# One-core linear attention, routed experts and a three-way maximum layer: the gate moved to the output's eviction, first row tiles transposed through two banks, filler matmuls at two boundaries, and the order of two products of the keys' norm

## The chip, the cores and the metric

The kernel runs on one core of one Trainium2 chip. The metric is the device time of one execution in microseconds (us); lower is better. The engines are TensorE (PE in the profile, with PEld for its weight loads), VectorE (DVE), ScalarE (ACT), GpSimd (POOL) and SyncE (SP, which here only starts DMAs).

## The reference

Three computations follow one another. All arithmetic is fp32.

```python
# attention: q, k, v are (4, 8, 768, 48), beta is (4, 8, 768)
k_n = k / (norm(k) + 1e-6)
for t in range(S):
    y[:, :, t] = einsum('bhd,bhde->bhe', q[:, :, t], state)
    v_old = einsum('bhde,bhd->bhe', state, k_n[:, :, t])
    state = state + beta_t * einsum('bhd,bhe->bhde', k_n[:, :, t], v_t - v_old)
x = y.transpose(0, 2, 1, 3).reshape(3072, 384)
# experts: one of 8 per row
e_idx = argmax(x @ w_gate); gate_w = softmax value of the chosen expert
out[row] = gate_w * sigmoid(x @ w_output_gate)[e_idx] * (relu(x @ w1[e]) @ w2[e])
# last layer
h = maximum(maximum(x @ w1, x @ w2), x @ w3);  out = h @ w_out
```

The combined factor of a row (the softmax value times the sigmoid) is positive. The last layer has no bias, so a positive factor on a row of its input can be applied to that row of its output.

## The kernel before, in words

There are three blocks of code. Each ends in a barrier of all engines, so no instruction of the next block runs before every engine has finished the one before.

**Attention and router.** The sequence is cut into chunks of 64 positions. Two streams (`st` 0 and 1) run half a step apart, and one step (12 in all) takes each of them through a pair of chunks. An order written out by hand sets what every engine issues: a step has 16 slots, and `walk` goes through the slots and calls `chain` (the work that carries the state from chunk to chunk, and the routing), `inv` (the inverse of a triangular matrix, per chunk) and `norm` (the key norms of the step that comes next). The tables `CHAIN`, `INV`, `PRE` and `NORM` give the slots. Engines are in order; semaphores tie them together.

The norm of the next step's keys is a row of short DVE operations, the parts 1 and 3 to 8 of `norm` (L586 to L607). Part 8 writes the inverse norm `nrm` (L607). Part 9 (L620) then makes `beta_k`, beta times the inverse norm, in four products of 64x8. POOL makes the normed keys `kn` (L664) from the raw keys and the same inverse norm, and waits for `inv_norm`, which part 8 raises. Behind part 9, DVE comes to `place` (L575), the routing product that reads what TensorE wrote to the stream's `chain` bank. TensorE's next `ks` product (L420) writes to that bank, so it waits for `place` (its semaphore is `routed`).

**Experts.** Rows stand sorted by expert in `x_sorted`. For each tile of 128 rows, `transpose_x` (L849) turns the loaded rows, ACT takes the high part and DVE the low part of the result (each operand is split in two fp32r parts, and a product takes three matmuls, helper `three`, L794), and the hidden and output products follow. Results go to `y_sorted`. The first tile needs its rows by DMA, the transposes, the high and the low part before the first product.

**Last layer.** There are 6 steps of 4 tiles (512 rows). POOL gathers rows from `y_sorted` in the original order (`gather`, L1114). DVE multiplies each gathered tile by its gate (`scale`, L1209) into one of two `scaled` buffers. TensorE transposes it into `o_bank[0]` (L1139), ACT takes the high part (L1176), DVE the low part (L1213). Three hidden products per 128 hidden columns (helper `three`, L1081) go to `h_bank`; ACT and DVE take their maximum (L1180, L1219, L1222) and split it (L1184, L1224). Then the output product fills `o_bank[t % 2]`, ACT copies it out (L1195) and SP stores it. For all steps but the first, the transposes stand between the hidden products of the step before. The first four tiles are transposed before the first step, one after the other, each waiting for the low part of the tile before (`x_lo`).

Of the kernel before, what the change touches and what calls it, by code (L numbers as in the profile page):

```python
# [16 lines left out]
P = 128  # L17
# [86 lines left out]
def attention_and_router(nc, ctx, sems, kt_in, kh, qh, vh, bh, cf_in, ch_in, wr_in, cf, ch, wr, routing, xs, ys, weights, w1, w2):  # L104
# [138 lines left out]
    NORM = {1: [0], 2: [1], 3: [2, 10], 5: [3], 6: [4], 7: [5], 8: [6, 13], 9: [7, 8, 9], 14: [11], 15: [12]}  # L243
# [80 lines left out]
    def _(pe):  # L324
# [146 lines left out]
        pe.matmul(bank[0][0][:, 0:E], ones16, counted[:], start=True, stop=True, skip_group_check=True).then_inc(totals_done, 1)  # L471

# [184 lines left out]
    def _(pool):  # L657
        def inv(k, par, st, what, lv):
            b = beta[:, 0, 2 * k + st, :]
            if what == "kn":  # L660
                pool.wait_ge(inv_norm, k + 1)
# [73 lines left out]
def experts(nc, ctx, sems, cf, routing, gate, slots, xs, ys, weights, w1, w2, w_in, w_out):  # L735
# [108 lines left out]
    def _(pe):  # L844
# [46 lines left out]

        transpose_x(0)
# [136 lines left out]
def last_layer(nc, ctx, sems, cf, gate, slots, ys, weights, out):  # L1029
# [14 lines left out]
    scaled = [sb(f"scaled{i}", [P, X]) for i in range(2)]  # L1044
# [16 lines left out]
    scaled_ready = sem("scaled_ready")  # L1061
# [16 lines left out]
    def three(pe, out, a, b, first, last):  # L1078
# [3 lines left out]
        return ins  # L1082

# [24 lines left out]
    def _(pool):  # L1108
        def gather(n, first):
            for t in range(NT):  # L1110
                if not first:
                    pool.wait_ge(scaled_ready, NT * n - NT + t + 1)
                    pool.sem_inc(passed_pool, 1)
# [16 lines left out]
    def _(pe):  # L1130
        def transpose_x(n, t, now=None):

            pe.wait_ge(scaled_ready, NT * n + t + 1)
            if t > 0:
                pe.wait_ge(x_lo, NT * n + t)
            elif now is not None:
                pe.wait_ge(o_out, NT * now + 1)
            for c in range(KX):
                ins = pe.transpose(o_bank[0][:, P * c:P * c + P], scaled[t % 2][:, P * c:P * c + P], ident)  # L1139
            ins.then_inc(x_done, 1)  # L1140
# [24 lines left out]

        for t in range(NT):
            transpose_x(0, t)
        for split in weights.last_lo:
            pe.wait_ge(split, 1)
# [3 lines left out]
    def _(act):  # L1173
        def x_part(n, t, par):
            act.wait_ge(x_done, NT * n + t + 1)
            act.copy(xt[par][0][:, :, P * t:P * t + P], o_bank[0][:, 0:X].rearrange("p (c t) -> p c t", c=KX)).then_inc(x_hi, 1)  # L1176
# [9 lines left out]
        def body(n, m, par, more):  # L1186
# [5 lines left out]
            for t in range(NT):  # L1192
                act.wait_ge(o_done, NT * n + t + 1)
                act.wait_ge(o_sent[t % 2], 8 * (NT * n + t - t % 2) + 1)
                act.copy(o_sb[t % 2][:], o_bank[t % 2][:, 0:X]).then_inc(o_out, 1)  # L1195
# [8 lines left out]
    def _(dve):  # L1204
        def scale(n, t):
            dve.wait_ge(rows_got[t], 16 * n + 16)
            if not (isinstance(n, int) and n == 0 and t < 2):
                dve.wait_ge(x_done, NT * n + t - 1)
            dve.tensor_scalar(scaled[t % 2][:], rows[t][:], gate[:, bass.ds(NT * n + t, 1)], None, ALU.mult).then_inc(scaled_ready, 1)  # L1209
# [121 lines left out]
```

## Time and profile before

| | us |
|---|---|
| median of 3 runs | 1111.56 |
| lowest and highest | 1108.06, 1112.52 |
| the profiled execution, its own time | 1108.98 |
| its span in the trace | 1107.3 |
| TensorE busy | 1026.3 |
| DVE, ACT, POOL busy | 509.7, 366.9, 335.4 |

The profiled execution is one more run. Its span counts from the first to the last recorded instruction; 1.7 us of its own time lie around it. The attention block runs to about 497 us of the span, the experts to about 777, the last layer to the end. The profile also gives the clock that TensorE was granted in a stretch, as a share of 2.4 GHz: 1.00 is 2.4 GHz and 0.50 is 1.2 GHz.

### The profile page before, as it was taken

What the parts mean: (1) busy time and instruction counts of PE and PEld (TensorE: products, weight loads), DVE (VectorE), ACT (ScalarE), POOL (GpSimd) and SP (SyncE); (2) the same over time, 40 slices, a digit from 0 to 9 for tenths busy, and PEclk for the clock granted to TensorE, in tenths of its full rate; (3) what the DMA queues carried; (4) which work ended last, traced back from release to release, by engine and by line L of the source; (5) the groups of instructions that cost most, each with busy time, mean ns of one, the idle gap of its engine ahead of it and who ended that gap; (6) DMA issues with size and microseconds to landing.
All of it is one profiled execution on the core that took longest, in us unless ns stands there. A gap on an engine that the chain in (4) does not pass through costs nothing. (4 is left out here: it accounts for less than half of the span.)

```text
span 1107.3 us, 30948 instructions
## 1 busy us (share of the span) xinstructions
PE 1026.3 (93%) x13260; PEld 895.4 (81%) x13260; DVE 509.7 (46%) x1085; ACT 366.9 (33%) x731; POOL 335.4 (30%) x251
## 2 busy tenths in 40 slices
PE   4898999999999999849999999999599999999998
PEld 3787888887888778737999999998488888888888
DVE  5575665666666655435444444433332323233221
ACT  1455544554555455412222222221121222122111
POOL 3444253435233422115352555525310001000000
PEclk9999998999999999958999999999699999999999
DMA  9212112121212111044344444223201010100000
GB/s 313 110 34 65 55 53 60 55 72 41 72 58 70 41 44 34 9 151 162 102 155 165 171 165 171 86 86 114 71 22 39 19 44 14 48 16 22 15 15 29
DMA packets 58056, 84.90 MB, mean 77 GB/s; under 512 B 28880, under 2 KB 52816, under 8 KB 55376
## 3 DMA queue, kind: packets, MB, share of 16 engines
q1 hardware_dynamic: 52272, 46.94, 13.5%
q0 software_dynamic: 5664, 36.18, 9.6%
q8 instruction: 98, 1.61, 0.6%
q14 instruction: 22, 0.18, 0.1%
HBM read 61.67 MB, written 21.43 MB: 75 GB/s over the span
## 5 line engine op out<-in xcount | busy, mean ns | idle before, releaser
L1081 PE MATMUL hb<-early,last_h 128*128 128x512 f32 x648 | 208.0, 402 | 1.2 <-DVE early L1213 1.2
L1081 PEld LDWEIGHTS hb<-early,last_h 128*128 128x128 f32 x648 | 121.7, 191 | 29.4 <-DVE early L1213 1.6
L1081 PE MATMUL hb<-early,last_l 128*128 128x512 f32 x324 | 129.3, 399 | 0.0
L1219 DVE TENSOR_TENSOR m<-hb,m 128x512 f32<-128x512 f32 x36 | 24.9, 692 | 132.3 <-PE hb L1081 132.3
L329 PEld LDWEIGHTS bank<-t,n_hi 64*64 64x64 f16 x2688 | 65.7, 111 | 23.6 <-issue 7.9
L540 DVE TENSOR_TENSOR p<-bank,cf 128x512 f16<-128x512 f32 x96 | 66.1, 689 | 32.2 <-PE bank L329 31.8
L329 PE MATMUL bank<-t,n_hi 64*64 64x64 f16 x2688 | 72.7, 195 | 4.9 <-issue 4.2
L1081 PE MATMUL ob<-wo_h,early 128*128 128x384 f32 x288 | 75.1, 339 | 0.0
L1081 PEld LDWEIGHTS hb<-early,last_l 128*128 128x128 f32 x324 | 61.6, 190 | 15.0
L1003 POOL TENSOR_TENSOR late<-w_raw,late 128x3072 fp32r<-128x3072 f32 x8 | 54.5, 6812 | 57.6 <-DVE late L943 57.3
L1114 POOL DMA_INDIRECT rows<-y_sorted,idx x24 | 23.0, 959 | 159.1 <-DVE scaled L1209 155.8
L537 DVE TENSOR_TENSOR t<-bank,cf 128x512 f16<-128x512 f32 x72 | 49.8, 692 | 45.7 <-PE bank L329 44.9
L912 ACT CAST ht_h<-ht_bank 128x512 fp32r<-128x512 f32 x56 | 32.9, 587 | 109.3 <-PE ht_bank L866 55.4
L489 ACT CAST t<-bank 128x512 f16<-128x512 f32 x96 | 56.3, 587 | 27.2 <-PE bank L329 25.0
L930 DVE TENSOR_TENSOR ht_l<-ht_bank,ht_h 128x512 fp32r<-128x512 f32 x56 | 38.7, 692 | 56.7 <-ACT ht_h L912 56.2
L794 PE MATMUL y_acc<-early,ht_h 128*128 128x384 f32 x240 | 63.8, 347 | 0.0
L794 PE MATMUL h_bank<-early,xt_h 128*128 128x512 f32 x180 | 58.5, 407 | 1.4 <-DVE xt_l L925 1.3
L420 PE MATMUL chain<-state,kq_t 128*128 128x96 f32 x384 | 54.8, 286 | 5.2 <-issue 5.0
L664 POOL TENSOR_TENSOR kn<-k_raw,nrm 128x384 f32<-128x384 f32 x24 | 20.1, 836 | 125.5 <-DVE nrm L607 125.2
L491 ACT CAST tt<-bank 128x512 f16<-128x512 f32 x96 | 57.0, 593 | 1.4 <-PE bank L329 1.3
L1003 POOL TENSOR_TENSOR early<-w_raw,early 128x3072 fp32r<-128x3072 f32 x6 | 40.9, 6810 | 52.7 <-DVE early L943 52.5
L794 PE MATMUL y_acc<-late,ht_h 128*128 128x384 f32 x208 | 55.2, 346 | 1.5 <-DVE ht_l L930 1.5
(163 smaller groups left out, 2194.7 us busy)
## 6 DMA issues: line engine op xcount, KB each, us to landing
w_raw<-w POOLq DMA_DIRECT2D x14, 1536.0 KB, 7.6
kq_t<-qh SPq DMA_DIRECT2D x24, 256.0 KB, 3.3
y_sorted<-y_sb SPq DMA_DIRECT2D x31, 192.0 KB, 1.9
x_in<-x_sorted SPq DMA_DIRECT2D x29, 192.0 KB, 2.8
k_raw<-kt_in SPq DMA_DIRECT2D x24, 192.0 KB, 3.2
v_in<-vh SPq DMA_DIRECT2D x24, 192.0 KB, 3.6
k_own<-kh SPq DMA_DIRECT2D x24, 192.0 KB, 3.4
out<-o_sb SPq DMA_DIRECT2D x24, 192.0 KB, 1.8
```

Of the source, the lines that this page charges most:

```text
L329: ins = pe.matmul(out[s, C * u:C * u + C], lhs(s, u), rhs(s, u), start=first and u == 0, stop=True, skip_group_check=True)
L420: ins = pe.matmul(out[:, W * p:W * p + W], kq_t[par][st][:, NP * e + p, :, :].rearrange("q a t -> q (a t)"), state[st][:, p].rearrange("q ...
L489: act.copy(t16[st][:], tb).then_inc(t_out[st], 1)
L491: act.copy(tt16[st][:], ttb).then_inc(tt_out[st], 1)
L537: dve.tensor_tensor(t16[st][:], pb, mask_of(None), ALU.mult).then_inc(jacobi_out[st], 1)
L540: dve.tensor_tensor(p16[st][:], pb, mask_of(lv), ALU.mult).then_inc(prod_out[st], 1)
L794: ins = pe.matmul(out, a[x], b[y], start=first and i == 0, stop=last and i == 2)
L912: act.copy(ht[0][:, 4 * n:4 * n + 4].rearrange("p c t -> p (c t)"), ht_bank[n][:, :]).then_inc(ht_hi[n], 1)
L930: dve.tensor_tensor(ht[1][:, 4 * n:4 * n + 4].rearrange("p c t -> p (c t)"), ht_bank[n][:, :], ht[0][:, 4 * n:4 * n + 4].rearrange("p c t ...
L1003: pool.tensor_tensor(splits[par][i][1], weights.flat_raw(i), splits[par][i][0], ALU.subtract).then_inc(weights.lo_ready[i], 1)
L1081: ins = pe.matmul(out, a[x], b[y], start=first and i == 0, stop=last and i == 2, skip_group_check=True)
L1219: dve.tensor_tensor(m1[f % 2][:], h_bank[f % 2][1][:, :], m0[f % 2][:], ALU.max).then_inc(m1_out, 1)
```

## The change

Four things change.

1. In the last layer, the gathered rows are transposed as they are. The gate is applied by DVE when it takes the output product out of its bank (`output`), in place of ACT's copy; `scale`, the `scaled` buffers and their semaphore are gone. POOL's next gather into a row buffer waits for the transposes of that buffer.
2. The first four tiles of the last layer are transposed through `o_bank[0]` and `o_bank[1]` in turn, so a tile waits for the low part of the tile two before it. The later tiles still use `o_bank[0]` alone.
3. TensorE gets matmuls whose results nobody reads: 12 of fp16 at the end of the attention block, 12 at the start of the experts, 12 at the start of the last layer and 3 after each of its first four transposed tiles. All have 512 columns.
4. In the attention, POOL's `kn` of every step but the first waits for `beta_k_ready` (raised by part 9) in place of `inv_norm`. The norm parts 3 to 9 stand one slot earlier in `NORM`.

```diff
-    NORM = {1: [0], 2: [1], 3: [2, 10], 5: [3], 6: [4], 7: [5], 8: [6, 13], 9: [7, 8, 9], 14: [11], 15: [12]}
+    NORM = {1: [0], 2: [1], 3: [2, 10], 4: [3], 5: [4], 6: [5], 7: [6], 8: [7, 8, 9, 13], 14: [11], 15: [12]}
...
         pe.matmul(bank[0][0][:, 0:E], ones16, counted[:], start=True, stop=True, skip_group_check=True).then_inc(totals_done, 1)
+        for _ in range(12):
+            pe.matmul(bank[1][2][:, :], tri16, flat(n_hi[1]), start=True, stop=True, skip_group_check=True)
...
             if what == "kn":
-                pool.wait_ge(inv_norm, k + 1)
+                if k >= 1:
+                    pool.wait_ge(beta_k_ready, k + 1)
+                else:
+                    pool.wait_ge(inv_norm, 1)
...
+        pe.wait_ge(weights.hi_ready[0], 1)
+        for _ in range(12):
+            pe.matmul(h_bank[1][:, :], w1s[0][0][:, 0, 0:P], w1s[0][0][:, 0, 0:512], start=True, stop=True, skip_group_check=True)
         transpose_x(0)
...
+    def x_bank(n, t):
+
+        return o_bank[t % 2 if isinstance(n, int) and n == 0 else 0]
...
-                    pool.wait_ge(scaled_ready, NT * n - NT + t + 1)
+                    pool.wait_ge(x_done, NT * n - NT + t + 1)
...
-            pe.wait_ge(scaled_ready, NT * n + t + 1)
-            if t > 0:
-                pe.wait_ge(x_lo, NT * n + t)
-            elif now is not None:
-                pe.wait_ge(o_out, NT * now + 1)
+            pe.wait_ge(rows_got[t], 16 * n + 16)
+            if now is None:
+                to = o_bank[t % 2]
+                if t >= 2:
+                    pe.wait_ge(x_lo, t - 1)
+            else:
+                to = o_bank[0]
+                if t > 0:
+                    pe.wait_ge(x_lo, NT * n + t)
+                else:
+                    pe.wait_ge(o_out, NT * now + 1)
             for c in range(KX):
-                ins = pe.transpose(o_bank[0][:, P * c:P * c + P], scaled[t % 2][:, P * c:P * c + P], ident)
+                ins = pe.transpose(to[:, P * c:P * c + P], rows[t][:, P * c:P * c + P], ident)
...
+        for split in weights.last_lo:
+            pe.wait_ge(split, 1)
+
+        def keep_warm(count):
+            for _ in range(count):
+                pe.matmul(h_bank[1][2][:, :], ws[0][0][:, 0, 0:P], ws[0][0][:, 0, 0:512], start=True, stop=True, skip_group_check=True)
+
+        keep_warm(12)
         for t in range(NT):
             transpose_x(0, t)
-        for split in weights.last_lo:
-            pe.wait_ge(split, 1)
+            keep_warm(3)
...
-            for t in range(NT):
-                act.wait_ge(o_done, NT * n + t + 1)
-                act.wait_ge(o_sent[t % 2], 8 * (NT * n + t - t % 2) + 1)
-                act.copy(o_sb[t % 2][:], o_bank[t % 2][:, 0:X]).then_inc(o_out, 1)
...
-        def scale(n, t):
-            dve.wait_ge(rows_got[t], 16 * n + 16)
-            if not (isinstance(n, int) and n == 0 and t < 2):
-                dve.wait_ge(x_done, NT * n + t - 1)
-            dve.tensor_scalar(scaled[t % 2][:], rows[t][:], gate[:, bass.ds(NT * n + t, 1)], None, ALU.mult).then_inc(scaled_ready, 1)
+        def output(n, t):
+            dve.wait_ge(o_done, NT * n + t + 1)
+            dve.wait_ge(o_sent[t % 2], 8 * (NT * n + t - t % 2) + 1)
+            dve.tensor_scalar(o_sb[t % 2][:], o_bank[t % 2][:, 0:X], gate[:, bass.ds(NT * n + t, 1)], None, ALU.mult).then_inc(o_out, 1)
...
             for f in range(KF):
-                if more and f < NT:
-                    scale(n + 1, f)
                 hidden(n, f)
                 if more and f < NT:
                     x_part(n + 1, f, 1 - par)
+            for t in range(NT):
+                output(n, t)
...
         for t in range(NT):
-            scale(0, t)
             x_part(0, t, 0)
```

## Rows read from the trace of the kernel before

**Rows 1.** The page: busy time of each engine; the last chain by line.
```profile
PE 1026.3 (93%) x13260; PEld 895.4 (81%) x13260; DVE 509.7 (46%) x1085; ACT 366.9 (33%) x731; POOL 335.4 (30%) x251
...
PE hb L1081 21%; PE ob L1081 7%; PE ob L1139 1%; DMA rows<-y_sorted,idx 0%; ACT early L1176 0%; DVE scaled L1209 0%; DVE early L1213 0%; ACT o_sb L1195 0%; POOL idx L1118 0%; POOLq L1302 0%
```

**Rows 2.** Windows: length, busy us (instructions) by engine, granted clock, DMA share, GB/s.
```profile
134.80:138.00 3.20, 3.20 (x47) 2.89 (x46) 2.86 (x12) 2.14 (x5) 0.84 (x2) 0.50 0.02 5
172.80:179.00 6.20, 6.20 (x102) 5.79 (x101) 3.75 (x16) 2.87 (x6) 2.33 (x4) 0.50 0.01 3
...
501.70:506.60 4.90, 4.90 (x12) 3.84 (x13) 3.15 (x10) 0.60 (x1) 0.78 (x1) 0.50 0.28 84
776.70:791.20 14.50, 3.60 (x12) 2.01 (x12) 3.94 (x12) 2.52 (x5) 7.99 (x10) 0.50 0.32 88
791.20:796.90 5.70, 5.66 (x13) 4.45 (x14) 2.89 (x2) 1.99 (x2) 2.17 (x3) 0.50 0.17 54
797.00:1104.50 307.50, 307.49 (x1452) 262.34 (x1450) 90.40 (x147) 62.27 (x114) 15.17 (x19) 1.00 0.08 25
```

**Rows 3.** Timeline of PE, attention: start, length, instruction, idle before and its releaser.
```profile
215.29 1.10 PE L420 MATMUL chain<-state,kq_t 128*128 128x96 f32 x8 [0.73 <-issue]
...
289.20 1.10 PE L420 MATMUL chain<-state,kq_t 128*128 128x96 f32 x8 [0.54 <-issue]
...
399.27 0.99 PE L420 MATMUL chain<-state,kq_t 128*128 128x96 f32 x7 [0.73 <-issue]
```

**Rows 4.** Timeline of DVE, the end of one step's norm.
```profile
249.37 0.17 DVE L598 TENSOR_TENSOR nrm<-nrm 128x16 f32<-128x16 f32 x1
...
249.78 0.25 DVE L607 RECIPROCAL nrm<-nrm 128x16 f32<-128x16 f32 x1
250.07 1.25 DVE L620 TENSOR_TENSOR beta_k<-nrm,beta 64x8 f32<-64x8 f32 x4
251.35 0.17 DVE L575 TENSOR_TENSOR place<-chain,chosen 128x8 f32<-128x8 f32 x1
```

**Rows 5.** Timeline, one step earlier, a narrow window: the second factor product, POOL's keys.
```profile
213.92 0.72 DVE L620 TENSOR_TENSOR beta_k<-nrm,beta 64x8 f32<-64x8 f32 x1
...
213.79 0.83 POOL L664 TENSOR_TENSOR kn<-k_raw,nrm 128x384 f32<-128x384 f32 x1 [11.46 <-DVE nrm L607]
```

**Rows 6.** Timelines of PE, DVE and SP at the first boundary.
```profile
490.71 0.17 PE L471 MATMUL bank<-counted,ch 128*128 128x8 f16 x1 [1.02 <-POOL counted L690]
499.54 0.90 PE L849 MATMUL xt_bank<-cf,x_in 128*128 128x128 f32 x3 [8.66 <-DMA x_in<-x_sorted]
...
497.26 0.38 DVE L989 MEMSET y_sb<- 128x384 f32 x1 [4.13 <-PEq L1297]
...
494.21 0.42 SPq L319 DMA_DIRECT2D x_sorted<-zeros  x1
```

**Rows 7.** The chain that ended last: two first groups of hidden products of the last layer.
```profile
791.24 9.12 PE hb L1081 x27
...
800.69 6.33 PE hb L1081 x27
```

**Rows 8.** Timelines of PE, DVE and POOL at the second boundary.
```profile
782.00 0.90 PE L1139 MATMUL ob<-cf,scaled 128*128 128x128 f32 x3 [7.92 <-DVE scaled L1209]
...
781.36 0.58 DVE L1209 TENSOR_SCALAR scaled<-rows,gate 128x384 f32<-128x384 f32 x1 [4.02 <-DMA rows<-y_sorted,idx]
...
782.07 0.95 POOL L1114 DMA_INDIRECT rows<-y_sorted,idx  x1 [0.30 <-issue]
785.48 0.19 POOL L1118 COPY idx<-slots 128x4 uint32 x1 [2.46 <-DMA rows<-y_sorted,idx]
```

**Rows 9.** Timelines: the last eviction, the nearest DVE eviction, DVE's idle in an output product.
```profile
1104.52 0.48 ACT L1195 COPY o_sb<-ob 128x384 f32<-128x384 f32 x1 [2.69 <-PE ob L1081]
...
774.21 0.56 DVE L936 COPY y_sb<-y_acc 128x384 f32<-128x384 f32 x1 [4.62 <-PE y_acc L794]
...
1058.15 0.69 DVE L1219 TENSOR_TENSOR m<-hb,m 128x512 f32<-128x512 f32 x1 [14.87 <-PE hb L1081]
```

More of the change, by code:

```diff
@@ L1043, in last_layer @@
     rows = [sb(f"rows{t}", [P, X]) for t in range(NT)]
-    scaled = [sb(f"scaled{i}", [P, X]) for i in range(2)]
     w1_early, w2_early = weights.split_early()
@@ L1060, in last_layer @@
     rows_got = [sem(f"rows_got{t}") for t in range(NT)]
-    scaled_ready = sem("scaled_ready")
     x_done = sem("x_done")
@@ L1175, in x_part @@
             act.wait_ge(x_done, NT * n + t + 1)
-            act.copy(xt[par][0][:, :, P * t:P * t + P], o_bank[0][:, 0:X].rearrange("p (c t) -> p c t", c=KX)).then_inc(x_hi, 1)
+            act.copy(xt[par][0][:, :, P * t:P * t + P], x_bank(n, t)[:, 0:X].rearrange("p (c t) -> p c t", c=KX)).then_inc(x_hi, 1)
         def hidden(n, f):
@@ L1204, in _ @@
     def _(dve):
-        def scale(n, t):
-            dve.wait_ge(rows_got[t], 16 * n + 16)
-            if not (isinstance(n, int) and n == 0 and t < 2):
-                dve.wait_ge(x_done, NT * n + t - 1)
-            dve.tensor_scalar(scaled[t % 2][:], rows[t][:], gate[:, bass.ds(NT * n + t, 1)], None, ALU.mult).then_inc(scaled_ready, 1)
+        def output(n, t):
+            dve.wait_ge(o_done, NT * n + t + 1)
+            dve.wait_ge(o_sent[t % 2], 8 * (NT * n + t - t % 2) + 1)
+            dve.tensor_scalar(o_sb[t % 2][:], o_bank[t % 2][:, 0:X], gate[:, bass.ds(NT * n + t, 1)], None, ALU.mult).then_inc(o_out, 1)
         def x_part(n, t, par):
             dve.wait_ge(x_hi, NT * n + t + 1)
-            dve.tensor_tensor(xt[par][1][:, :, P * t:P * t + P], o_bank[0][:, 0:X].rearrange("p (c t) -> p c t", c=KX),
+            dve.tensor_tensor(xt[par][1][:, :, P * t:P * t + P], x_bank(n, t)[:, 0:X].rearrange("p (c t) -> p c t", c=KX),
                               xt[par][0][:, :, P * t:P * t + P], ALU.subtract).then_inc(x_lo, 1)
```

## The prediction

> **What bounds the kernel now.** I read the page first. TensorE is busy 93% of the span and no other engine half of it, and the last chain is TensorE alone with small pieces of the last layer's start around it [rows 1]. So time can only come from TensorE's own idle stretches and from stretches in which it ran slowly. The windows show both. From 797.0 to 1104.5 TensorE has no gap and its clock is 1.00, so nothing in the body of the last layer can be gained by relieving another engine there; it can only be lost. At either boundary the clock is at 0.50 (1.2 GHz) and TensorE mostly waits; it comes back to 1.00 only after 4.9 us of unbroken products at the first boundary and 5.7 us at the second [rows 2]. Then I read TensorE's timeline in the attention for its idle times. One is regular: 0.73 us ahead of the `ks` product of stream 1, in six steps from 215.3 to 399.3 (five of 0.73, one of 0.54) [rows 3]. The DVE rows just ahead tell why: the tail of the norm, then the four `beta_k` products, then `place`, and `ks` starts about 0.1 us after `place` ends [rows 4]. The narrow window shows that the second `beta_k` product took 0.72 us and ended with POOL's `kn`, which had begun 0.13 us before it; the last three took 1.1 us together, so the two others 0.18 each [rows 4, 5].
>
> **The attention.** If `kn` starts only behind `beta_k`, the four products take 4 x 0.18 = 0.7 us and not 1.25, which brings `place` 0.55 us forward. Norm part 6 (0.17 us, 0.2 with its gap) leaves the stretch ahead of `place` for slot 7, where DVE has idle time: another 0.2. Parts 7 to 9 move over a slot in which DVE has nothing else, so their order on DVE is unchanged; parts 3 to 5 move into idle stretches between short PSUM reads. Together 0.75 us, against a wait of 0.73: the wait goes in all six steps, 5 x 0.73 + 0.54 = 4.2 us [rows 3, 4]. What is late next: the gram product waits for ACT's `kq_t`, which ends about when the shifted gram could start, and everything behind it follows TensorE. The added wait on POOL holds back `kn` by 0.7 us, and behind it the counting, the scatter of rows and the mask; `kn` is read only in the next slot 0, and POOL had been idle 11.5 us before it [rows 5], so this costs nothing. In the steps before 215 the wait is hidden under pauses of TensorE or under the slow clock. Bounds: 0, if another wait takes its place, to 5.7 us, if two earlier steps gain 0.73 as well. I take 4.2.
>
> Two stretches of the attention ran at 0.50 without being idle, 3.2 and 6.2 us long [rows 2]. At full clock they would have taken half, so they cost 1.6 + 3.1 = 4.7 us. Nothing in the change touches these places, and I cannot tell from one trace whether they come in every execution; they go into the range.
>
> **The first boundary.** The 12 fillers at the end of the attention start behind the 0.17 us product at 490.71. There is no row of a 128x512 fp16 matmul; the nearest are fp32r ones of this size, 12 in 4.9 us at the slow clock [rows 2] and 27 in 6.33 us, 0.234 each, at the full one [rows 7]. So the fillers run 490.9 to about 496.0 at the slow clock. SP issues the last DMA of the block at 494.21 and the experts start at 497.1 to 497.3 [rows 6], so that DMA's landing hides them, with about 1 us to spare. If they ran over, each would cost 0.41 us.
>
> The second 12 start at about 497.3. Before, TensorE's first transposes stood at 499.54, when the rows had come [rows 6], and the first product at 501.7. At the full clock the fillers take 2.8 us and end at 500.1; transposes of 0.5 (half of the 0.90 at the slow clock) and the high and low parts (1.1 with their gaps) bring the first product to 501.7, where it was, now at the full clock: a gain of half of 4.9, 2.4 us [rows 2]. At the slow clock they take 4.9 to 5.1, end at 502.4 and put the first product at 504.5, a loss of 2.8 us; with the clock back by then, 2.8 - 2.4 = 0.4 us of loss. Which one depends on when the clock rises. After 4.9 to 5.7 us of work, as in the two rows, it would rise at 495.8 to 496.6, right about when the first fillers end. I take the case that a third of the second batch is still slow (4 x 0.2 us late): -2.4 + 0.8 = -1.6 us, with bounds of -2.4 and +2.8.
>
> A rule of the Trainium skill bears on this. "TensorE: Matmul & The Clock Gate", section "HAM oscillation — how this bites in real kernels", says that bursts of matmuls with waits between them can meet the slow clock each time anew; the same page's Part 1 has the point of the rise vary from run to run. By it, two batches with 1.3 us between them need not hold the clock, and this boundary would be the loss of rival 2. The rows here have no two bursts of this length with such a gap, so they neither agree nor disagree.
>
> **The second boundary.** Before, the rows of the first tile came at 781.34, DVE scaled them, and then four tiles went one after the other through one bank; the first product stood at 791.24 [rows 7, 8]. From 782.00 that is 9.2 us. In the new order 12 fillers start at about 777.3, just when the clock has fallen, and end at about 782.3 (12 x 0.42); the clock has risen by then or shortly after (777.3 + 4.9 to 5.7). The rows are there, no scaling stands between, so the first transposes start at 782.3, not 782.0: 0.3 us later. Each tile then takes 0.5 for its transposes and 0.7 for three fillers: tile 1 at 783.5, tile 2 at 784.7 (its bank is free: the low part of tile 0 ends at 783.9), tile 3 at 785.9. The fourth gather is issued at 782.07 and POOL sees all four landed at 785.48 [rows 8], so tile 3 could not start before 785.4 anyhow. Its transposes, high and low part end at 787.5: the first product comes 3.7 us earlier. The last three fillers end at 787.1 and are hidden. The first 27 products took 9.12 us against 6.33 at the full clock [rows 7], another 2.8. Sum: -6.5 us. Bounds: -7.0 (tile 3 the moment it lands, at 785.4) and -3.0 (clock back only at 785: all four tiles slow, about 2 us later, and part of the 2.8 lost). I take -6.3. With the first product at 787.5, ACT's and DVE's split of `w_out` ends in time for the first maxima, as it stands behind the same parts as before.
>
> **The evictions.** The 24 `scale` products (0.41 to 0.58 us each) leave DVE and 24 evictions come in. The nearest row is DVE's copy of a 128x384 bank, 0.56 us against ACT's 0.48 [rows 9]. DVE idles 14.9 us between its last work of a step and the next [rows 9], and an output tile takes 12.7 / 4 = 3.2 us of TensorE with two banks in turn, so 0.56 us is hidden there and costs nothing; without that cover it would be 24 x 0.56 = 13.4 us. Only the last stands in the open: +0.1 us. POOL's gathers now wait for the transposes instead of the scaling, one product group later, with more than 20 us until the rows are used: nothing.
>
> **Sum.** -4.2 - 1.6 - 6.3 + 0.1 = -12.0 us. The profiled execution took 1108.98 in its own time (its span 1107.3 and 1.7 around it): 1097.0. It was 2.6 us faster than the median of the runs, 1111.56, so the same change from the median would be 1099.6. I take about the middle, 1098.
>
> **The rivals.**
> 1. In the attention another wait takes the place of the one removed, or `beta_k` is held by something else: 0 instead of -4.2. For it: a hand-made order with little slack, and ACT's `kq_t` right behind. Against it: the wait after `place` is 0.1 us, so it alone released `ks`. About 1102.
> 2. The first boundary turns to a loss, the second batch slow throughout: +1.5 instead of -1.6. About 1101.
> 3. At the second boundary the clock comes late: -3.0 instead of -6.3. About 1101.5.
> 4. Slower: DVE's eviction is exposed. DVE is in order, so if `output` holds up the maxima of the next step, or a bank comes free too late, TensorE waits each time. At 0.56 us for all 24 that is +13.4: 1.4 us over before, about 1112. It decides from 0.5 us exposed per eviction on. Against it stands the idle time of 14.9 us.
>
> **How the numbers follow.** The forecast as summed has a chance of 0.60, with a range of its own of 1094 to 1101 (the two slow stretches of the attention gone or doubled make most of it). Rival 1 has 0.13, rival 2 0.12, rival 3 0.11, rival 4 0.04. The range of 1091 to 1105 runs from the forecast without the slow stretches (1097.0 - 4.7 = 1092.3, less the 1 us of the bounds) to two rivals at once. A measurement of this kernel can tell about 0.5%, 5.6 us, from no change: that is 1106. Rivals 1 to 3 alone all stay below it. Two of them together with an unlucky execution, and most of rival 4, fall within it: 0.05. Slower, the rest of rival 4 (evictions longer than 0.56): 0.015. Faster: 0.935.
>
> **What would show it.** The attention: the four `beta_k` products at 0.7 us, `kn` starting behind them, and no idle time before L420 in the regular steps. The first boundary: the attention's last DMA, not TensorE, still ahead of the barrier; the clock at 1.00 when the first product starts, at 501.7 or a little later counted from the same barrier. The second: the transposes 1.2 us apart, the first product about 10.3 us after the barrier and not 14.1, 27 products in 6.33 us. The last layer: from the first product on as long as before, no gap on TensorE. A prediction too low would show TensorE waiting for `o_out` or `m2_out`, or fillers at 0.43 us right up to the first transposes of the experts.

## The result, and the profile after

The changed kernel takes 1096.72 us (median of 4 runs, 1095.28 to 1098.27). The kernel before, run in turn with it, takes 1109.81 us. The ratio is 0.989, with a 95% interval of 0.9856 to 0.9924: the kernel is 1.1% faster. The forecast was 1098.0, within 1091 to 1105.

The profiled execution of the changed kernel has a span of 1094.7 us, against 1107.3: 12.6 us less. Laid side by side, from mark to mark, the two profiled executions differ like this. A mark is the start of a row in a timeline of TensorE, or the end of a product; the start of a block is where DVE's first instruction behind the barrier stands.

| stretch | before, us | after, us | difference | predicted |
|---|---|---|---|---|
| start to the attention's last counting product (L471) | 490.71 | 486.93 | -3.78 | -4.2 |
| L471 to the end of the first expert tile's hidden products | 17.56 | 15.36 | -2.20 | -1.6 |
| from there to the experts' last product | 265.81 | 265.87 | +0.06 | 0 |
| to the start of the last layer's block | 3.12 | 3.12 | 0 | 0 |
| block start to the end of the first 27 hidden products | 23.16 | 16.28 | -6.88 | -6.3 |
| the rest of the last layer | 306.94 | 307.14 | +0.20 | +0.1 |

The page of the changed kernel, busy time and last chain, to lay beside [rows 1]:

```profile
PE 1034.8 (95%) x13308; PEld 899.7 (82%) x13308; DVE 507.0 (46%) x1085; ACT 355.3 (32%) x707; POOL 335.3 (31%) x251
...
PE hb L1087 21%; PE ob L1087 7%; PE ob L1155 1%; PE hb L1187 1%; DVE o_sb L1227 0%; DVE early L1231 0%; ACT early L1199 0%
```

ACT has lost 24 instructions and 11.6 us of work, TensorE has gained 48 matmuls and 8.5 us. Neither figure says where the time went; that is seen at the places themselves. First DVE's timeline at the end of a norm, and its last eviction. This answers to [rows 4, 9]:

```profile
322.55 0.25 DVE L609 RECIPROCAL nrm<-nrm 128x16 f32<-128x16 f32 x1
322.84 0.69 DVE L622 TENSOR_TENSOR beta_k<-nrm,beta 64x8 f32<-64x8 f32 x4
323.56 0.17 DVE L577 TENSOR_TENSOR place<-chain,chosen 128x8 f32<-128x8 f32 x1
...
357.96 0.25 DVE L609 RECIPROCAL nrm<-nrm 128x16 f32<-128x16 f32 x1
...
1091.72 0.62 DVE L1227 TENSOR_SCALAR o_sb<-ob,gate 128x384 f32<-128x384 f32 x1 [2.55 <-PE ob L1087]
```

The four `beta_k` products take 0.69 us where they took 1.25. The two reciprocals are one step apart: 35.41 us, where the same pair stood 36.17 apart. POOL's timeline, with `kn` behind `beta_k` (which, of that step, began at 215.38), the first of the four gathers, and the copy that waits for all four:

```profile
216.14 0.83 POOL L669 TENSOR_TENSOR kn<-k_raw,nrm 128x384 f32<-128x384 f32 x1 [11.41 <-DVE beta_k L622]
...
772.31 1.02 POOL L1124 DMA_INDIRECT rows<-y_sorted,idx  x1 [0.59 <-POOL idx L1128]
...
779.58 0.18 POOL L1128 COPY idx<-slots 128x4 uint32 x1 [2.48 <-DMA rows<-y_sorted,idx]
```

TensorE's timeline at the two boundaries, beside [rows 6, 8]:

```profile
486.93 0.17 PE L471 MATMUL bank<-counted,ch 128*128 128x8 f16 x1 [1.01 <-POOL counted L695]
486.96 4.85 PE L473 MATMUL bank<-n_hi,ch 128*128 128x512 f16 x12
493.38 2.98 PE L899 MATMUL h_bank<-early 128*128 128x512 f32 x12 [1.57 <-PEq L1314]
...
498.00 0.70 PE L799 MATMUL h_bank<-early,xt_h 128*128 128x512 f32 x2 [1.25 <-DVE xt_l L933]
...
771.40 4.46 PE L1187 MATMUL hb<-last_h 128*128 128x512 f32 x12 [3.24 <-PEq L1319]
775.70 0.49 PE L1155 MATMUL ob<-cf,rows 128*128 128x128 f32 x3
...
779.25 0.55 PE L1155 MATMUL ob<-cf,rows 128*128 128x128 f32 x3
```

The chain that ended last, with the first two groups of hidden products, beside [rows 7]:

```profile
780.96 6.60 PE hb L1087 x27
787.88 6.32 PE hb L1087 x27
```

And the windows, columns as in [rows 2]: the first expert tile, the start of the last layer in two parts, its body, and a stretch of the attention.

```profile
493.00:503.00 10.00, 8.37 (x40) 6.62 (x40) 5.75 (x17) 3.03 (x6) 0.87 (x1) 1.00 0.37 120
771.40:776.00 4.60, 4.60 (x16) 3.65 (x16) 0.03 (x2) 0.00 (x0) 3.12 (x4) 0.66 0.27 78
776.00:781.00 5.00, 4.53 (x24) 2.76 (x22) 2.23 (x4) 2.61 (x5) 1.48 (x3) 1.00 0.29 87
788.00:1092.00 304.00, 303.68 (x1434) 259.26 (x1432) 97.50 (x151) 51.13 (x91) 16.01 (x20) 1.00 0.08 26
139.50:150.00 10.50, 10.23 (x126) 9.00 (x127) 3.76 (x8) 2.69 (x6) 5.64 (x5) 0.51 0.18 51
```

The reader sees full clock throughout the first expert tile, the clock risen before the gathered rows are turned, and a last layer still without gaps. The last row is the one thing that has not changed: 10.5 us of the attention still run at half clock while TensorE is busy for 10.23 of them.

One caution goes ahead of all experiments. Eleven variants were run, and the changed kernel once more; each profile is one execution, and executions of one kernel lie far apart (the kernel before: 1101.6 to 1116.5 us over all its runs; the variants: 3 to 15 us from end to end). One execution of `b2_second_batch_only` (4951 us) and one of `d4_changed_again` (2467 us) took several times as long, for no reason on record; the ratios leave them out, and without the latter the median of `d4_changed_again` is 1097.83 us and not 1099.34. A part worth 2 us can't be told from the medians of whole runs. The ratios are given, but the verdicts are read from stretches between marks, which repeat far better: from the transposes that follow the first 27 hidden products (0.16 us ahead of their modelled end) to the end of the span, the last layer takes 307.2 to 307.3 us in every profile of the changed kernel's kind that keeps the evictions as they are.

### The profile page after: what moved, and what is told of

The parts are those of the page before. It is cut to its first block and busy times, and to the rows that moved or that the text cites. A ratio compares the mean times of both kernels' runs of the same rounds, so it can differ in the third digit from the quotient of the medians.

```text
span 1094.7 us, 30983 instructions
## 1 busy us (share of the span) xinstructions
PE 1034.8 (95%) x13308; PEld 899.7 (82%) x13308; DVE 507.0 (46%) x1085; ACT 355.3 (32%) x707; POOL 335.3 (31%) x251
## 3 DMA queue, kind: packets, MB, share of 16 engines
q0 software_dynamic: 5664, 36.18, 9.6%
## 5 line engine op out<-in xcount | busy, mean ns | idle before, releaser
L439 PE MATMUL chain<-z,n_kb_a 128*128 128x96 f32 x384 | 56.2, 291 | 1.1 <-issue 1.1
```

Source lines behind the costliest of these rows:

```text
L439: ins = pe.matmul(out[:, W * p:W * p + W], n_kb_a[par][st][:, NP * e + p, 1:3, :].rearrange("q a t -> q (a t)"), z[st][:, p].rearrange("q ...
```

## The experiments

Every variant below is an edit of the changed kernel.

### The attention: undone, and its two halves

`a1_attention_undone` puts the old table and the old wait back. `b1_slots_only` keeps the new table and puts back the wait alone.

```diff
-    NORM = {1: [0], 2: [1], 3: [2, 10], 4: [3], 5: [4], 6: [5], 7: [6], 8: [7, 8, 9, 13], 14: [11], 15: [12]}
+    NORM = {1: [0], 2: [1], 3: [2, 10], 5: [3], 6: [4], 7: [5], 8: [6, 13], 9: [7, 8, 9], 14: [11], 15: [12]}   # a1 only
...
             if what == "kn":
-                if k >= 1:
-                    pool.wait_ge(beta_k_ready, k + 1)
-                else:
-                    pool.wait_ge(inv_norm, 1)
+                pool.wait_ge(inv_norm, k + 1)                                                                  # a1 and b1
```

> The changed kernel with the attention edits alone taken back (the old slots of the norm, and the keys' product waiting for the inverse norm again). My theory (the factor products were held by POOL's key product, and the place product behind them released the next ks product): the four beta_k products take 1.25 us again, the idle time of 0.73 us ahead of the ks product is back in six steps, and the run is 3.8 to 4.2 us longer than the changed kernel, all of it before the product of the totals. Rival (the attention got shorter because fewer or shorter slow-clock stretches fell in it, not by the wait): the attention is as long as in the changed kernel once the time at the 0.50 clock is taken out, so 0 to 1 us.

> The changed kernel with the keys' product waiting for the inverse norm again, as before, and the new slots of the norm kept. The clean steps of the attention were 36.17 us long before and 35.41 with the change. My theory (0.55 us from the order against POOL, 0.2 from norm part 6 leaving the stretch): the beta_k products take 1.25 us, the clean steps 35.9 to 36.0 us, about 3 us more than the changed kernel over the steps in which it counts. Rival (the slots do it all, the products' length is hidden): 35.4 us per clean step, 0 us.

Measured: a1 takes 1099.4 us (4 runs), a ratio to the kernel before of 0.9897 (0.9851 to 0.9943); b1 1098.79 (10 runs), 0.9915 (0.9881 to 0.9948). DVE's timeline of a1:

```profile
325.26 0.25 DVE L609 RECIPROCAL nrm<-nrm 128x16 f32<-128x16 f32 x1
325.55 1.25 DVE L622 TENSOR_TENSOR beta_k<-nrm,beta 64x8 f32<-64x8 f32 x4
...
361.44 0.25 DVE L609 RECIPROCAL nrm<-nrm 128x16 f32<-128x16 f32 x1
```

DVE's and TensorE's timelines of b1:

```profile
322.98 0.25 DVE L609 RECIPROCAL nrm<-nrm 128x16 f32<-128x16 f32 x1
323.26 1.25 DVE L622 TENSOR_TENSOR beta_k<-nrm,beta 64x8 f32<-64x8 f32 x4
...
358.94 0.25 DVE L609 RECIPROCAL nrm<-nrm 128x16 f32<-128x16 f32 x1
...
360.78 0.99 PE L420 MATMUL chain<-state,kq_t 128*128 128x96 f32 x7 [0.50 <-issue]
```

The same kind of step takes 36.18 us in a1 (361.44 - 325.26), 35.96 in b1 and 35.41 in the changed kernel, which all three have in steps without a pause of TensorE. So the new slots bring 0.21 of the 0.76 and the order against POOL the other 0.55, the sizes the prediction gave them (0.2 and 0.55). `beta_k` goes back to 1.25 us whenever `kn` may start beside it. TensorE's wait ahead of L420 is 0.73, 0.50 and none. Summed over the attention, the idle time ahead of L420 was 5.0 us in the kernel before (9 times), 4.7 in a1 (8), 1.6 in the changed kernel (twice, 1.25 of it in one pause at 139.77) and 5.6 in b1 (11). So the wait in b1 is shorter but comes more often, and this sum doesn't rank the two halves; the length of a step does.

The whole stretch to L471 doesn't show this well. It was 486.93 us in the changed kernel's first profile, and with the same attention 481.00 to 494.14 in the profiles of other variants. The medians of a1 and of the changed kernel differ by 2.7 us in the right direction, inside their scatter, and not by the 3.8 to 4.2 that were expected. The rival's own measure doesn't decide either. With half of the time at the 0.50 clock taken out, the stretch to L471 is 475.6 us in a1 and 475.4 in the changed kernel, which is where the rival put it; but the same figure lies between 470.4 and 479.5 in the other profiles with the changed attention.

A shorter stretch tells more. The five steps between the reciprocals at 213.46 and 397.44 us of the kernel before take 183.98 us. They take 183.03 in a1, 181.16 in b1, 179.53 in the changed kernel, and 177.84 to 183.15 in the ten other profiles with its attention; the median of these eleven is 179.53. The forecast for them was 3.5 us less (five of the six waits, 4 x 0.73 + 0.54). The median is 3.5 below a1 and 4.5 below the kernel before, which is about that, and ten of the eleven lie below a1 and the kernel before. With one profile each of a1, b1 and the kernel before, it is not measured to a microsecond.

### The first boundary: no fillers, half of them, more of them

`a2_no_fillers_first` takes away both batches, `b2_second_batch_only` the first one; `d2_first_16` makes the first one 16; `d4_changed_again` is the changed kernel once more.

```diff
         pe.matmul(bank[0][0][:, 0:E], ones16, counted[:], start=True, stop=True, skip_group_check=True).then_inc(totals_done, 1)
-        for _ in range(12):                        # a2, b2: both lines gone; d2: range(16)
-            pe.matmul(bank[1][2][:, :], tri16, flat(n_hi[1]), start=True, stop=True, skip_group_check=True)
...
-        for _ in range(12):                        # a2: both lines gone
-            pe.matmul(h_bank[1][:, :], w1s[0][0][:, 0, 0:P], w1s[0][0][:, 0, 0:512], start=True, stop=True, skip_group_check=True)
         transpose_x(0)
```

> The changed kernel without both filler batches at the first boundary. My theory (the clock alone): from the totals product to the last hidden product of the first expert tile it takes 17.5 us as before the change, not 15.4; the clock comes back about 5 us after the first hidden product; +2.2 us in all. Rival (the gain at this boundary came from something else that moved earlier): 15.4 to 16 us without fillers too.

> The changed kernel without the first batch of 12 fillers, the second kept. My theory (a batch that starts at the 0.50 clock holds up the transposes by more than it gives back): the 12 fillers take 4.5 to 5 us, the first hidden product stands 13.0 to 13.6 us behind the totals product (11.1 in the changed kernel, 11.0 before), and the first expert tile's hidden products end after 17.3 to 17.9 us, as before the change: no gain at this boundary. Rival (the second batch alone carries the gain): 15.4 to 16.9 us.

> The changed kernel with 16 and not 12 fillers in the first batch. Theory (the clock rises under the first batch and falls again while TensorE waits for the barrier, if that wait is over about 2 us; four more fillers shorten it by 0.9 us): the second batch runs at the full clock, and the first tile's hidden products end 15.3 to 15.6 us behind the totals product, not 16.8 as in four of the six executions profiled so far. Rival (the fall does not hang on the length of the gap): 16.7 to 16.9 again.

> The changed kernel once more, for the scatter between executions beside the other three and a second profile. Expected: 1094 to 1100 us in the median; clean attention steps of 35.4 us; the first boundary 15.4 or 16.8 us; the second 9.6 to 9.7 us to the first product.

Measured: a2 1100.02 us (9 runs), ratio 0.9911 (0.9885 to 0.9938); b2 1101.39 (9 runs), 0.9937 (0.9907 to 0.9968); d2 1097.97 (6 runs), 0.9907 (0.987 to 0.9944); d4 1099.34 (6 runs), 0.9901 (0.9874 to 0.9928).

In a2 TensorE idles 9.17 us up to the transposes. TensorE's timeline of b2 and of d2, their batches:

```profile
499.00 4.74 PE L897 MATMUL h_bank<-early 128*128 128x512 f32 x12 [6.27 <-PEq L1312]
```

```profile
487.76 5.55 PE L473 MATMUL bank<-n_hi,ch 128*128 128x512 f16 x16
494.17 3.01 PE L899 MATMUL h_bank<-early 128*128 128x512 f32 x12 [0.86 <-PEq L1314]
```

TensorE's timeline of d4, which is the changed kernel unchanged:

```profile
494.14 0.17 PE L471 MATMUL bank<-counted,ch 128*128 128x8 f16 x1 [1.01 <-POOL counted L695]
494.17 4.44 PE L473 MATMUL bank<-n_hi,ch 128*128 128x512 f16 x12
500.58 4.58 PE L899 MATMUL h_bank<-early 128*128 128x512 f32 x12 [1.97 <-PEq L1314]
504.99 0.49 PE L854 MATMUL xt_bank<-cf,x_in 128*128 128x128 f32 x3
506.73 0.70 PE L799 MATMUL h_bank<-early,xt_h 128*128 128x512 f32 x2 [1.25 <-DVE xt_l L933]
```

Its windows over the second batch and behind it:

```profile
500.58:505.00 4.42, 4.42 (x13) 3.44 (x14) 1.38 (x5) 1.73 (x3) 0.00 (x0) 0.61 0.54 180
...
500.58:501.00 0.42, 0.42 (x2) 0.38 (x3) 0.32 (x2) 0.42 (x1) 0.00 (x0) 1.00 0.00 0
501.10:504.40 3.30, 3.30 (x9) 2.55 (x8) 0.96 (x4) 1.21 (x3) 0.00 (x0) 0.50 0.71 237
...
505.00:509.00 4.00, 2.75 (x14) 2.12 (x13) 2.19 (x11) 0.48 (x1) 0.00 (x0) 1.00 0.32 102
```

Here the second batch takes 4.58 us in place of 2.98. The granted clock was still 1.00 through the 1.97 us between the batches and for the first 0.4 us of the second one; then it was 0.50, and it was 1.00 again before the transposes. Eight profiles have the two batches of 12 (the variants that edit other places have them too). They fall in two groups, and the other counts stand beside them. The first three columns are lengths in us; the last is counted from L471.

| executions | first batch takes | idle before the second | second batch takes | end of the first tile's hidden products |
|---|---|---|---|---|
| 12 and 12: after, b1, d3 | 4.85 to 5.28 | 1.14 to 1.57 | 2.98 to 3.01 | 15.32 to 15.39 |
| 12 and 12: a1, a3, a4, c1, d4 | 4.04 to 4.47 | 1.94 to 2.38 | 4.4 to 4.6 | 16.73 to 16.90 |
| 16 and 12: d2 | 5.55 | 0.86 | 3.01 | 15.54 |
| 0 and 12: b2 | | 6.27 | 4.74 | 17.05 |
| none: before, a2 | | | | 17.56, 18.35 |

The second batch starts 6.43 to 6.44 us behind L471 in all eight. So a first batch that meets an early rise of the clock is over sooner, the idle time behind it is longer, and the second batch is slow: the clock fell 0.2 to 0.4 us before it began in a1 and a3, and 0.3 to 0.5 us after in a4, c1 and d4. Even then the stretch is 0.7 to 0.8 us shorter than it was in the kernel before (and about 1.5 shorter than in a2), because the clock is back for the first real products. Both batches at their best bring 2.2.

Two of these expectations were not met, and a third proves little. a2 was to take 17.5 us and took 18.35; its transposes wait 0.5 us longer for their rows than in the kernel before, and the rest is a later rise of the clock. So two single profiles without fillers lie 0.8 us apart, and every gain against either has that uncertainty. b2, at 17.05, lies between its two theories (17.3 to 17.9, and 15.4 to 16.9): the second batch alone is worth 0.5 us against the kernel before and 1.3 against a2, which is not settled. d2 came out as its theory said (15.54), but three of the eight profiles with 12 fillers did as well, so one profile does not show that 16 are better.

### The second boundary: no fillers, one bank

```diff
-        keep_warm(12)                              # a3
         for t in range(NT):
             transpose_x(0, t)
-            keep_warm(3)                           # a3
...
-        return o_bank[t % 2 if isinstance(n, int) and n == 0 else 0]
+        return o_bank[0]                           # a4
...
-                to = o_bank[t % 2]
-                if t >= 2:
-                    pe.wait_ge(x_lo, t - 1)
+                to = o_bank[0]                     # a4
+                if t >= 1:
+                    pe.wait_ge(x_lo, t)
```

> The changed kernel without the 12 fillers and the 4 times 3 fillers of the last layer. Theory A (the tiles are paced by the gathers, which land 1.27 us apart, and the fillers only fix the clock): the first product comes 9.7 to 10.1 us after the block begins, as with fillers, and the first 27 products take 9.1 us and not 6.6; +2.5 to +3 us. Theory B (my prediction: the fillers set the pace of the tiles): the first product comes up to 1 us earlier without them, so +1.5 to +2 us.

> The changed kernel with the first four tiles transposed through one bank (each waits for the low part of the tile before), all fillers kept. Theory A (gathers land 1.27 us apart; a tile through one bank takes about 1.7 us at the full clock): the first product comes about 1.5 us later, +1.5 us. Rival (removing the scaling alone was enough, the landing of the fourth gather binds in both): 0 to 0.5 us.

Measured: a3 1099.27 us (5 runs), ratio 0.9905 (0.9869 to 0.994); a4 1100.68 (10 runs), 0.9929 (0.9891 to 0.9968). TensorE's timeline of a3:

```profile
777.80 0.87 PE L1155 MATMUL ob<-cf,rows 128*128 128x128 f32 x3 [7.37 <-DMA rows<-y_sorted,idx]
...
781.44 0.90 PE L1155 MATMUL ob<-cf,rows 128*128 128x128 f32 x3 [0.28 <-DMA rows<-y_sorted,idx]
```

The chain of a3, its first group of products:

```profile
783.50 8.39 PE hb L1087 x27
```

TensorE's timeline of a4, its last tile:

```profile
782.65 0.52 PE L1155 MATMUL ob<-cf,rows 128*128 128x128 f32 x3 [0.55 <-DVE early L1231]
```

And the kernel before, its second tile, on DVE and TensorE:

```profile
783.45 0.56 DVE L1213 TENSOR_TENSOR early<-ob,early 128x384 fp32r<-128x384 f32 x1 [1.50 <-ACT early L1176]
783.93 0.41 DVE L1209 TENSOR_SCALAR scaled<-rows,gate 128x384 f32<-128x384 f32 x1
784.39 0.90 PE L1139 MATMUL ob<-cf,scaled 128*128 128x128 f32 x3 [1.49 <-DVE scaled L1209]
```

| behind the block's start, us | tiles start | first product | end of the 27 products |
|---|---|---|---|
| before | 4.80, 7.19, 9.58, 11.98 | 14.04 | 23.16 |
| after | 4.42, 5.46, 6.70, 7.97 | 9.68 | 16.28 |
| a3, no fillers | 4.25, 5.45, 6.70, 7.89 | 9.95 | 18.34 |
| a4, one bank | 4.53, 6.28, 8.05, 9.83 | 11.51 | 18.09 |

Without fillers each tile waits for its own rows and starts when they land, within 0.2 us of the times with fillers; the transposes take 0.90 us and not 0.55, and the first product is only 0.27 us later. So with two banks POOL's gathers set the pace, one each 1.27 us, landing 3.1 us after their issue. The fillers give the clock and nothing else: 8.39 us for 27 products against 6.60 (I had expected 9.1), and 0.27 ahead of them, 2.1 together. With one bank a tile waits 0.55 us for the low part of the tile before, the tiles are 1.78 us apart, and the first product is 1.83 later. What remains of the 6.88 is 3.0 us, if the parts simply add: the scaling that no longer stands between a gather and its transposes, and what the parts bring only together. It was not tried by itself. The lines of the kernel before show what it did there: DVE took the scaling of a tile only behind the low part of the tile before, so the transposes waited for that low part and then 0.41 us of scaling, and a tile took 2.39 us.

### The evictions, doubled

`c1_double_eviction` gives DVE 24 more evictions of the same size, into spare buffers.

```diff
             dve.wait_ge(o_sent[t % 2], 8 * (NT * n + t - t % 2) + 1)
+            dve.tensor_scalar(spare[t % 2][:], o_bank[t % 2][:, 0:X], gate[:, bass.ds(NT * n + t, 1)], None, ALU.mult)
             dve.tensor_scalar(o_sb[t % 2][:], o_bank[t % 2][:, 0:X], gate[:, bass.ds(NT * n + t, 1)], None, ALU.mult).then_inc(o_out, 1)
```

> The changed kernel with every output eviction of the last layer done twice by DVE, the first time into a spare buffer: 24 more products of 0.56 us. My theory (DVE idles there and two banks alternate every 3.2 us): TensorE's products follow without a gap, and only the last eviction shows, +0.6 us. Rival (the evictions are exposed): up to 24 times 0.56, +13 us.

Measured: 1098.31 us (10 runs), ratio 0.9923 (0.9895 to 0.995). DVE's timeline at its end:

```profile
1087.19 0.62 DVE L1228 TENSOR_SCALAR spare<-ob,gate 128x384 f32<-128x384 f32 x1 [2.03 <-PE ob L1088]
1087.73 0.61 DVE L1229 TENSOR_SCALAR o_sb<-ob,gate 128x384 f32<-128x384 f32 x1
```

Its window over the same length of the last layer as that of the changed kernel above:

```profile
784.00:1088.00 304.00, 303.16 (x1432) 258.83 (x1430) 109.72 (x174) 50.53 (x90) 15.98 (x20) 1.00 0.08 26
```

DVE is 12.2 us busier and TensorE 0.5 less busy in 304 (both windows end 2.7 us before the span does, and behind the last product c1 has one eviction more to do). From the transposes behind the first 27 products the last layer takes 307.83 us, against 307.30, and the second eviction of the last tile alone makes 0.54 of that (1087.73 - 1087.19). The other 23 cost nothing, so 23 evictions at half that length cost nothing either.

### Three tries at more

`c2_tail_fillers` puts 24 more fillers into the gaps of the attention's last step and makes the batch behind L471 22. `d3_early_gather` lets the first gathers read `slots` itself, ahead of the copy to `idx`. `d1_combined` has both, with 18 behind L471.

```diff
+        AHEAD = {("rank", 0, 0): 5, ("z", 1, 1): 3, ("up", 1, 1): 3, ("yt", 0, 1): 2, ("lg", 0, 1): 2, ("rank", 0, 1): 5}   # c2, d1
+            if k == STEPS - 1:
+                fill(AHEAD.get((what, e, st), 0))
...
+        fill(4)
         pe.wait_ge(counted_ready, TILES + 1)
...
-        for _ in range(12):
+        for _ in range(22):                        # d1: 18
...
+                at = slots if first else idx       # d3, d1
-        numbers(0)
         gather(0, True)
+        numbers(0)
```

> The changed kernel with 24 more fillers of 128x512 fp16 among the last chain products of the attention (2 to 5 ahead of each product that waits for DVE or ACT there), and 22 and not 12 behind the totals product. There the clock falls to 0.50 at about 474 and TensorE is busy 6.2 of the last 10.9 us. Theory A (the clock falls because of the waits, and the waits are long enough for the fillers): the clock stays at 1.00 up to the experts, the stretch from 474 to the totals product is 3 us shorter, and the second batch finds the full clock every time: -3 to -4 us in all. Theory B (each filler runs over into the chain, which is bound by latency): the chain gains what the clock gives and loses as much to fillers that are still running: 0, or 1 to 2 us slower.

> The changed kernel with the fillers among the last chain products of the attention (as in the run before), 18 fillers behind the totals product, and the first four gathers of the last layer reading their row numbers from the table itself, so that they are issued ahead of the copy of the numbers. Expected against the changed kernel: 2 to 2.5 us in the attention's tail, 0 to 1.5 at the first boundary, 0.3 to 0.8 at the second: 3 to 4 us less, about 1093 in the median if the scatter between executions lets it be seen. Rival (the gain in the tail is given back at the barrier, which stood 0.9 us later in the run before): 1 to 2 us less.

> The changed kernel with the first four gathers of the last layer issued ahead of the copy of the row numbers, 0.8 us earlier. Theory A (the landing of the fourth gather sets the fourth tile): the first product comes 8.9 us behind the start of the block, not 9.6 to 9.7. Theory B (the 12 fillers and the three per tile set the pace once the gathers are earlier): 9.2 to 9.6 us.

Measured: c2 1097.35 us (10 runs), ratio 0.9906 (0.9869 to 0.9943); d1 1098.15 (8 runs), 0.9925 (0.9897 to 0.9952); d3 1099.05 (4 runs), 0.9907 (0.9875 to 0.9938). None is shown to be faster than the changed kernel. TensorE's timeline of c2:

```profile
487.63 0.17 PE L480 MATMUL bank<-counted,ch 128*128 128x8 f16 x1
487.66 4.91 PE L482 MATMUL bank<-n_hi,ch 128*128 128x512 f16 x22
494.98 3.00 PE L908 MATMUL h_bank<-early 128*128 128x512 f32 x12 [2.41 <-PEq L1323]
```

TensorE's timeline of d1, its second batch:

```profile
491.93 4.57 PE L908 MATMUL h_bank<-early 128*128 128x512 f32 x12 [3.49 <-PEq L1324]
```

In c2 the clock is 1.00 from 473 us on, through the end of the attention and the 2.41 us between the batches, and from the last `rank` product of stream 0 to L471 it takes 11.10 us, against 13.47 in the changed kernel: 2.4 gained. But the experts' block then starts later behind L471, and the hidden products end at 16.22 in place of 15.36: 0.9 is given back. That leaves 1.5 of the 3 to 4 us expected. SP's waits of the changed kernel and of c2 show where (time in all, times, longest):

```profile
SPq L1314 <- PEq L1314: 0.2, 1, 0.2
```

```profile
SPq L1323 <- PEq L1323: 1.1, 1, 1.1
```

SP comes to the barrier and waits 1.1 us for TensorE's sequencer. In d1 the tail is again fast (10.82), the batch is over after 4.04 us, TensorE idles 3.49, the clock falls 0.9 us after the second batch has begun, and the hidden products end at 18.01: all given back, where the rival still had 1 to 2 us left. In d3 the first gather was issued 0.98 us behind the block's start in place of 1.03. The copy that it no longer needs was not what it waited for, so this run tests neither theory of the pace.

## Why the prediction was right

**The attention (-4.2).** Right in mechanism and in size per step: `beta_k` 0.69 against 0.7 foretold, `kn` behind it, the step 0.76 us shorter against 0.75, and 0.55 and 0.2 for its two halves, each by an experiment. Over the whole attention the two profiles differ by 3.78, but other profiles of the same attention lie 6 to 7 us to either side, so that this is so near to 4.2 is luck, and the total is not shown to a microsecond. What stands behind it is the length of a step and of five steps in a row (183.98 us before, 179.53 in the median of eleven profiles). That speaks against rival 1: no other wait came in the place. The cause of the held `beta_k` is one that the Trainium skill names ("SBUF — State Buffer", section "Who interferes with whom"): a VectorE instruction with two SBUF inputs and a GpSimd instruction that reads SBUF shut each other out, and the first to issue holds the port for its whole length. By that rule, the traces agree: 0.72 us for a product of 0.18 that met `kn`, and 0.17 us at most for each in steps 2 to 12 of the changed kernel. The first step, which keeps the old wait, shows the counterpart: there the four still take 2.89 us.

**The first boundary (-1.6).** The profile of the changed kernel shows -2.20, the others with the same batches -0.66 to -2.24 against the kernel before; the mean of the eight is 16.28, a gain of 1.3. The size came out near by luck: -1.6 lies between two outcomes, and neither is the one that I described. I took the clock to be slow for the first third of the second batch, 0.8 us late in all. What happens is one of two things: it rises late in the first batch and holds, or it rises early, the batch shrinks, the pause grows to about 2 us and the second batch is slow but for its first half microsecond at most. That second case is rival 2's mechanism, and it came in five of eight profiles, so 0.12 was far too low for it. Its price was wrong the other way: not +1.5 but -0.7. I had the slow second batch end 11.7 us behind L471 and the first product at 13.8. In d4 the batch ends at 10.9 (the block starts sooner than I took, and 12 products take 4.6 and not 5.1), the clock is back for the transposes, and the first product stands at 12.59. The rule of the Trainium skill that I weighed ("TensorE: Matmul & The Clock Gate", section "HAM oscillation — how this bites in real kernels") tells of bursts with waits of some 3 to 5 us between them, each of which meets the slow clock anew. I stretched it: a wait of 1.3 us is not one of those, so the section didn't speak for rival 2 as I had it. These profiles show the slow clock behind waits of 1.94 to 2.38 us, shorter than the section's, and there the measurement decides.

**The second boundary (-6.3).** The result was -6.88, within the bounds of -3.0 and -7.0: 4.36 from the first product (3.7 foretold) and 2.52 from the 27 products (2.8). The step that was off is the pace. I let the 12 fillers last to 5.1 us behind the block's start and the groups of three set the distance. The fillers end at 4.42, because the clock rises some 3.1 us after they begin (0.66 granted over 4.60 us is 0.50 for 3.1 and 1.00 for 1.5), where I took 4.9 at the least, and from then on each tile starts as its rows land: a3 has nearly the same times without any filler. So the first product stood at 9.68 and not at 10.3. The 27 products took 6.60, not 6.33. Rival 3 did not come in the changed kernel. In d2 it half did: there the 12 fillers took 5.46 us, and the 27 products ended 0.8 us later than usual.

**The evictions (+0.1).** Right: DVE's eviction takes 0.62 us (I had 0.56), ACT's took 0.48, and only the last one shows. Rival 4 is refuted by c1.

**The total.** The terms added to -12.0; the profiled spans differ by 12.6 and the medians by 13.1. That they agree so well is in part luck: executions of the changed kernel alone lie between 1094.95 and 1105.00 us, and when it was run again with the kernel before beside it, the difference was 11.1 us (1097.83 against 1108.89). The largest share of the uncertainty was rightly put on the slow stretches of the attention, but it was put too small. The two of the first profile were no fixture: over all profiles the time at half clock ahead of 470 us (from windows of 1 us: the sum of twice what each granted clock lacks to 1.00) adds up to between 3.4 and 21.9 us. It was 10.2 us in both the kernel before and the changed one, so it takes no part in the difference between these two.

## What to carry to other kernels

Read a stretched small operation for its neighbour: four products at 1.25 us that should take 0.7 meant that another engine's operation started beside them, and the cure was to order it behind them, at no cost, since it had slack. Filler matmuls are worth what the following real products gain from the clock. A fixed number of them shrinks when the clock rises early, so the pause that they leave up to a barrier is longest just then. When a serial chain through one buffer is widened, look for the next source of its pace (here the issue of the gathers, 1.27 us apart) before adding anything to the gaps; and where single executions scatter by more than the effect, compare stretches between marks, not totals.

## What the runs showed that I had not expected

- Stretches at half clock in the attention while TensorE is all but fully busy (10.23 of 10.5 us in the window above) differ from execution to execution, 3.4 to 21.9 us in all, and with them the time of a run. Most begin in or just behind pauses of 0.5 to 1.7 us within straight groups of matmuls, for which the trace names no releaser; but most such pauses are not followed by one (the changed kernel has 13 of 0.45 us or more between 60 and 472 us, and one such stretch there). What makes the pauses, and which of them cost the clock, is open, and it is the largest thing left: half of such a stretch is lost.
- Around the same kind of pause at the first boundary the clock held four times (idle 0.86 to 1.57 us: the changed kernel, b1, d3, d2) and once at 2.41 (c2), and fell five times (1.94 to 2.38 with 12 and 12) and once at 3.49 (d1). In four of these six it fell only 0.3 to 0.9 us after the next batch had begun. The length of the pause alone does not tell which it will be: c2 held at 2.41, where a1 fell at 2.38. And in the profiles with 12 and 12 a longer pause always goes with an earlier rise of the clock, so the two are not told apart.
- With more fillers ahead of the barrier the next block starts 0.9 to 1.1 us later (c2 and d1), with SP waiting for TensorE's sequencer (1.1 us against 0.2), although TensorE's last filler had ended before. Why the sequencer is late is open.
- The transposes of 128x128, 0.90 us for three at half clock, take 0.49 to 0.55 at the full one, and no profile shows the clock falling among transposes and fillers in turn.
